# Attention and two expert layers on one core: another order of the transfers that SyncE issues in a head

## The chip, the cores and the metric

The kernel runs on 1 core of one Trainium2 chip. The metric is the device time of one execution in microseconds. The kernel before takes 752.03 us (median of 3 runs, 750.96 to 754.53).

## What is computed

All arrays are f32. Three stages follow each other; the output of one is the input of the next.

```python
# 1. attention, 16 heads (2 x 8) of 768 positions x 64
q_bucket = sum((q @ proj > 0) * 2**arange(6)); k_bucket likewise
mask     = q_bucket[:, None] == k_bucket[None, :]
scores   = where(mask, q @ k.T / 8, -1e9); scores -= max(scores, -1)
attn     = exp(scores); attn /= sum(attn, -1) + 1e-9
x        = attn @ v                        # 1536 tokens x 512 after the heads are joined
# 2. dense layer, w_in 512 x 2048, w_out 2048 x 512
h = x @ w_in; g = where(h > 0, h, exp(min(h, 0)) - 1); x = g @ w_out
# 3. 8 experts (512 x 1024, 1024 x 512), one for each token; tokens with x @ w_skip <= 0 pass unchanged
out = x + gate * (relu(x @ w1[e]) @ w2[e])
```

## The kernel before, in words

Precision comes from splitting each f32 operand into a rounded high part and the rest (`hi`, `lo`; `p_hi`, `p_lo`; `W[:, j, 0..3, :]`), so that most products take three matmuls or two stacked ones.

**A head on TensorE.** `scores(h, s)` (L1187) makes six tiles of transposed scores, s = 0 to 5; four tiles later `weighted(n, b)` (L1199) multiplies the probabilities of tile n with v. Between them PE prepares the next heads, by the plan of `head_units` (L59): in head h the six row maxima `MAX` of head h+1 (L1180), at s = 2 the transposes `T` of q and k of head h+2 (L1164), at s = 3 the transpose of the maxima, at s = 4 the hash bits. `scores(h, 0)` waits for `neg_copied` (L1192): the row of minus maxima of head h must have been copied by DMA from `minus_max` into row 96 of `q_hi_rows_T` (`copy_minus_maxima`, L342).

**SyncE (SP)** issues nearly all transfers from one in-order queue, and its waits hold up all that is behind them. The loop at L386 runs over the heads h:

- `load_qk(h+3)` (two transfers of 192 KB) and `load_v(h+2)` (192 KB); the first waits for the transposes of head h+1, the second for `v_ready` (POOL's `low_of_v`, L504);
- in odd heads from 3: `store_rden` (12 inverse sums per partition to `den_rows` in HBM, L355), `load_w` of one dense tile (two transfers of 256 KB, L321), and `load_rden` (L361), which waits until the store has landed and reads the inverse sums back as `rden_rows`, each of 2 rows of 3 KB spread over 64 partitions, 384 KB;
- `copy_rows(h+2)` (four copies of 64 partitions x 3 KB within SBUF, L327; waits for `hi_done` of head h+2, that is ACT's `round_qk` behind the transposes), `copy_minus_maxima(h+1)`, `copy_low_rows(h+2)` (two more copies);
- in even heads from 2: `load_den` (L347), the sums of the pair of heads before.

The broadcast is written with the two rows as its leading dimension:

```python
sp.dma_start(rden_rows[:, :], den_rows[2 * pair:2 * pair + 2, :].unsqueeze(1).broadcast_to([2, D, S]))
```

**GpSimd (POOL)** makes the low parts of four tiles of six (`low_probs`, L512), the low part of v, in even heads from 4 `normalise(h // 2 - 2)` (L532: waits for `rden_loaded`, two multiplications into `attn_T`), in odd heads 3 to 9 `split_w` of one dense tile (L521), in heads 11 and 13 half of `split_x` (L543). All in program order: per head low_probs of 6h-2, 6h-1 and 6h, then normalise or the splits, then low_probs of 6h+3 (L571), then low_of_v. **VectorE (DVE)** has the other two tiles, the row maxima, `inverse_den` (L875) and, in the dense layer, `low_of_w` (L918). **ScalarE (ACT)** has the exponentials, `high_probs`, `outputs` (L687) and `high_of_w` (L721).

**Dense layer.** Four blocks of 384 tokens; each goes over 16 tiles j of `W` (`up`, L1238; `down`, L1251). Block 0 runs while the later tiles are still loaded and split. The tiles of `W` overlay the attention buffers: 4 to 7 are free after the last scores, 8 to 12 after `od_ready` of head 15, 13 to 15 after the last normalise (`xt_ready`). So SP (L405 to L416) loads 4 to 7, then `load_den(7)`, tile 8, `store_rden(7)`, `load_rden(7)`, tiles 9 to 12, and then 13 to 15. Four semaphores `w_loaded` go round: tile j waits until tile j-4 has been split (`w_done` of j-3).

Of the kernel before, what the change touches and what calls it, by code (L numbers as in the profile page):

```python
# [15 lines left out]
P = 128  # L16
B, NH, S, D = 2, 8, 768, 64
HEADS = B * NH
# [25 lines left out]


EARLY = 4

# [28 lines left out]
def build(nc, q, k, v, proj, w_in, w_out, w_skip, w_gate, w1, w2, out, y_rows):  # L78
    ctx = ExitStack()
    with ctx:  # L80
# [14 lines left out]
        def sem(name):  # L95
            return ctx.enter_context(nc.semaphore(name))
# [4 lines left out]
        w_raw = [sb(f"w_raw{j}", [P, 4, 512], F32, at=W_at + j * W_TILE)[0] for j in range(FT)]  # L101
# [134 lines left out]
        s_ = {n: sem(n) for n in names}  # L236
        qk_loaded = [sem(f"qk_loaded{u}") for u in range(2)]
        v_loaded = [sem(f"v_loaded{u}") for u in range(2)]
        rows_copied = [sem(f"rows_copied{i}") for i in range(3)]
        w_loaded = [sem(f"w_loaded{i}") for i in range(4)]  # L240
        e_loaded = [sem(f"expert_loaded{i}") for i in range(4)]
        gathered = [sem(f"rows_gathered{i}") for i in range(EXPERTS)]
        scattered = [sem(f"rows_scattered{i}") for i in range(2)]
# [4 lines left out]
        w_in_v = w_in.rearrange("(c p) (j f) -> j p c f", p=P, f=P)  # L248
# [60 lines left out]
        def _(sp):  # L309
            def load_qk(h):  # L310
                if h >= 2:
                    sp.wait_ge(s_["tq_done"], h - 1)
                for i, x in enumerate((q_h, k_h)):
                    sp.dma_start(qk_nat[h % 2][:, :, i, :], x[h]).then_inc(qk_loaded[h % 2], 16)

            def load_v(h):
                if h >= 2:
                    sp.wait_ge(s_["v_ready"], h - 1)
                sp.dma_start(v_nat[h % 2][:, :, :], v_h[h]).then_inc(v_loaded[h % 2], 16)

            def load_w(j):  # L321
                if j >= 4:
                    sp.wait_ge(s_["w_done"], j - 3)
                sp.dma_start(w_raw[j][:, 1, :].rearrange("p (c f) -> p c f", f=P), w_in_v[j]).then_inc(w_loaded[j % 4], 16)
                sp.dma_start(w_raw[j][:, 3, :], w_out_v[j]).then_inc(w_loaded[j % 4], 16)

            def copy_rows(h):  # L327
                i = h % 3
# [26 lines left out]
            def store_rden(pair):  # L355
                sp.wait_ge(s_["rden_ready"], pair + 1)
                for u in range(2):
                    sp.dma_start(den_rows[2 * pair + u].rearrange("(p t) -> p t", t=QT), rden[:, u * QT:(u + 1) * QT])\
                        .then_inc(s_["rden_stored"], 16)

            def load_rden(pair):  # L361
                sp.wait_ge(s_["rden_stored"], 32 * (pair + 1))
                if pair:
                    sp.wait_ge(s_["xt_ready"], pair)
                sp.dma_start(rden_rows[:, :], den_rows[2 * pair:2 * pair + 2, :].unsqueeze(1).broadcast_to([2, D, S]))\
                    .then_inc(s_["rden_loaded"], 16)
# [17 lines left out]
            copy_minus_maxima(0)  # L384

            for h in range(HEADS):  # L386
                if h + 3 < HEADS:
                    load_qk(h + 3)
                if h + 2 < HEADS:
                    load_v(h + 2)  # L390
                if h % 2 and h >= 3:
                    store_rden(h // 2 - 1)
                    if h // 2 <= EARLY:
                        load_w(h // 2 - 1)
                    load_rden(h // 2 - 1)
                if h + 2 < HEADS:
                    copy_rows(h + 2)
                if h + 1 < HEADS:
                    copy_minus_maxima(h + 1)
                if h + 2 < HEADS:  # L400
                    copy_low_rows(h + 2)
                if h % 2 == 0 and h:
                    load_den(h // 2 - 1)

            sp.wait_ge(s_["st_done"], QT * HEADS)  # L405
            for j in range(EARLY, EARLY + 4):
                load_w(j)
            load_den(PAIRS - 1)
            load_w(EARLY + 4)
            store_rden(PAIRS - 1)  # L410
            load_rden(PAIRS - 1)
            for j in range(EARLY + 5, 13):
                load_w(j)
            sp.wait_ge(s_["xt_ready"], PAIRS)
            for j in range(13, FT):
                load_w(j)  # L416
# [49 lines left out]
        def _(pool):  # L466
# [53 lines left out]

            def split_w(j):  # L521

                pool.wait_ge(w_loaded[j % 4], 32 * (j // 4 + 1))
                for i, raw in enumerate((1, 3)):
                    pool.tensor_scalar(W[:, j, 2 * i, :], w_raw[j][:, raw, :], 1.0, 1.0, ALU.mult, ALU.mult)\
                        .then_inc(s_["w_step"], 1)
                    pool.wait_ge(s_["w_step"], 2 * j + i + 1)
                    low = pool.tensor_tensor(W[:, j, 2 * i + 1, :], w_raw[j][:, raw, :], W[:, j, 2 * i, :].bitcast(F32),
                                             ALU.subtract)
                low.then_inc(s_["w_done"], 1)  # L530
# [29 lines left out]
            for h in range(HEADS):  # L560
                if h:
                    low_probs(QT * h - 2)
                    low_probs(QT * h - 1)
                low_probs(QT * h)
                if h % 2 == 0 and h >= 4:
                    normalise(h // 2 - 2, *low_ready(QT * h))
                if h % 2 and h >= 3 and h // 2 <= EARLY:
                    split_w(h // 2 - 1)
                if h in (11, 13):
                    split_x(0, ((h - 11) // 2,))  # L570
                low_probs(QT * h + 3)  # L571
                if 0 < h < HEADS - 1:
                    low_of_v(h + 1)
# [78 lines left out]
        def _(act):  # L652
# [67 lines left out]

            def high_of_w(j):  # L721

                act.wait_ge(w_loaded[j % 4], 32 * (j // 4 + 1))
                act.activation(W[:, j, 0:4:2, :], w_raw[j][:, 1:4:2, :], ACT.Copy).then_inc(s_["w_high"], 1)

            def g_high(n, j):
# [73 lines left out]
        def _(dve):  # L800
# [134 lines left out]
            def block_body(n):  # L935
                first = isinstance(n, int)
                for j in range(FT):
                    dve.wait_ge(s_["e_ready"], n * FT + (j + 1))

                    reached(dve, "gl_ready", n * FT + (j - 1))  # L940
                    dve.scalar_tensor_tensor(gb[:, j % 2, :], e_neg[:, j % 2, :], -1.0, banks[:, j % 2, 0:BN],  # L941
                                             ALU.add, ALU.max).then_inc(s_["g_ready"], 1)
                    if first and j == 1:
                        dve.wait_ge(s_["pv_done"], QT * HEADS)
                    if j:
                        g_low(n, j - 1)
                    elif not first:
                        g_low(n - 1, FT - 1)
                    if first and EARLY <= j + 2 < FT:
                        low_of_w(j + 2)  # L950
                    if first and j == 4:
                        inverse_den(PAIRS - 1)
                    if not first:
                        if j == 2:
                            y_T_copy(n - 1, 0)
                            y_T_copy(n - 1, 1)
                        elif j == 3:
                            y_T_copy(n - 1, 2)
                        elif j == 4:
                            logits_copy(n - 1)  # L960
# [476 lines left out]
```

## Time and profile before

| | before |
|---|---|
| median of 3 runs | 752.03 us (750.96 to 754.53) |
| profiled execution, its own time | 749.8 us |
| its span, first to last instruction | 747.8 us |
| mean granted TensorE clock | 0.944 of full |
| PE busy | 658.4 us (88%) |
| DVE, ACT, POOL busy | 344.3, 328.2, 252.1 us |
| head 4 to the end of attention | 96 to 327 us |
| dense layer | 327 to 610 us |
| experts | 636 to 748 us |

PE is TensorE's matmuls, PEld its weight loads, SPq SyncE's queue as issuer of DMAs. An engine's idle time before an instruction is shown with what released it. The clock column of a window is the share of 2.4 GHz that was granted; 0.50 is the lower level, 1.2 GHz.

### The profile page before, as it was taken

What the parts mean: (1) busy time and instruction counts of PE and PEld (TensorE: products, weight loads), DVE (VectorE), ACT (ScalarE), POOL (GpSimd) and SP (SyncE); (2) the same over time, 40 slices, a digit from 0 to 9 for tenths busy, and PEclk for the clock granted to TensorE, in tenths of its full rate; (3) what the DMA queues carried; (4) which work ended last, traced back from release to release, by engine and by line L of the source; (5) the groups of instructions that cost most, each with busy time, mean ns of one, the idle gap of its engine ahead of it and who ended that gap; (6) DMA issues with size and microseconds to landing.
All of it is one profiled execution on the core that took longest, in us unless ns stands there. A gap on an engine that the chain in (4) does not pass through costs nothing.

```text
span 747.8 us, 9851 instructions
## 1 busy us (share of the span) xinstructions
PE 658.4 (88%) x3632; PEld 610.3 (82%) x3632; DVE 344.3 (46%) x495; ACT 328.2 (44%) x505; POOL 252.1 (34%) x204
## 2 busy tenths in 40 slices
PE   4799688695959696999799999999999994999996
PEld 3699688695959595998699999999999983999986
DVE  6766656372737374425452322322232225654642
ACT  2367557373737464756354233333333331234340
POOL 4044747464657465672203000300001202711211
PEclk9999989797979798999899999999999996899999
DMA  7344626163453523041500100200036675599300
GB/s 177 87 122 122 150 65 156 40 170 69 130 110 97 116 76 85 3 134 53 166 29 34 53 1 0 84 0 0 0 140 224 241 267 209 192 372 354 134 11 22
DMA packets 68151, 84.04 MB, mean 112 GB/s; under 512 B 34356, under 2 KB 44692, under 8 KB 68112
## 3 DMA queue, kind: packets, MB, share of 16 engines
q1 hardware_dynamic: 66832, 79.88, 36.2%
q0 software_dynamic: 1280, 3.65, 1.4%
q8 instruction: 24, 0.39, 0.2%
q14 instruction: 15, 0.12, 0.1%
HBM read 56.64 MB, written 8.44 MB: 87 GB/s over the span
## 4 chain that ended last, share of the span: by engine, by line
PE 73%; DMA 15%; DVE 4%; SPq 3%; issue 2%; ACT 2%; POOL 0%; POOLq 0%; DVEq 0%; ACTq 0%
PE banks L1247 17%; PE banks L1258 16%; DMA q_hi_rows_T<-minus_max 9%; PE banks L1371 8%; PE banks L1386 6%; PE banks L1180 4%; PE banks L1195 4%; PE banks L1196 3%; PE banks L1211 3%; PE banks L1212 3%; PE banks L1213 3%; SPq L334 2%; DVE row_max L848 2%; DMA w_raw<-in_moe_w_out 2%; DMA y_rows<-y 2%
## 5 line engine op out<-in xcount | busy, mean ns | idle before, releaser
L1247 PE MATMUL banks<-x_hi,w_split 128*128 (+1 forms) x512 | 143.1, 340 | 4.1 <-DVE w_split L920 4.1
L517 POOL TENSOR_TENSOR probs_lo<-probs,probs_hi 128x768 fp32r<-128x768 f32 x64 | 107.6, 1691 | 110.5 <-ACT probs_hi L684 107.3
L848 DVE TENSOR_REDUCE row_max<-banks 128x1 f32<-128x768 f32 x96 | 88.5, 957 | 110.0 <-PE banks L1180 110.0
L676 ACT ACTIVATE probs<-banks 128x768 f32<-128x768 f32 x96 | 77.9, 811 | 121.4 <-PE banks L1196 120.5
L941 DVE SCALAR_TENSOR_TENSOR g<-exp_min_h,banks 128x384 f32<-128x384 f32 x64 | 35.5, 554 | 191.0 <-ACT exp_min_h L746 191.0
L1258 PE MATMUL banks<-w_split,g_hi 128*128 128x512 f32 x384 | 121.0, 396 | 0.1
L1195 PE MATMUL banks<-q_lo_hi_T,k_hi_lo_T 128*128 128x384 f32 x192 | 72.4, 377 | 54.6 <-DMA q_hi_rows_T<-minus_max 46.6
L743 ACT ACTIVATE exp_min_h<-banks 128x384 f32<-128x384 f32 x64 | 31.5, 492 | 169.8 <-PE banks L1247 169.8
L1247 PEld LDWEIGHTS banks<-x_hi,w_split 128*128 128x128 f32 x512 | 94.7, 190 | 7.1 <-issue 4.5
L1195 PEld LDWEIGHTS banks<-q_lo_hi_T,k_hi_lo_T 128*128 128x128 f32 x192 | 38.6, 201 | 61.5 <-issue 48.9
L1247 PE MATMUL banks<-x_lo,w_split 128*128 (+1 forms) x256 | 86.7, 339 | 0.0
L1258 PEld LDWEIGHTS banks<-w_split,g_hi 128*128 128x128 f32 x384 | 71.2, 189 | 12.4 <-DVE g_lo L915 0.5
L684 ACT ACTIVATE probs_hi<-probs 128x768 fp32r<-128x768 f32 x96 | 80.4, 838 | 0.0
L1258 PE MATMUL banks<-w_split,g_lo 128*128 128x512 f32 x192 | 76.2, 397 | 0.0
L1211 PE MATMUL banks<-probs_hi,v_hi_ones 128*128 128x386 f32 x192 | 67.3, 350 | 1.8 <-ACT o_and_den L695 1.8
L1196 PE MATMUL banks<-q_hi_rows_T,k_hi_rows_T 128*128 128x384 f32 x192 | 68.2, 355 | 0.0
L1212 PE MATMUL banks<-probs_lo,v_hi_ones 128*128 128x386 f32 x192 | 67.1, 350 | 0.0
L1213 PE MATMUL banks<-probs_hi,v_lo_zeros 128*128 128x386 f32 x192 | 67.0, 349 | 0.0
L1371 PEld LDWEIGHTS banks<-x_T,expert_w 128*128 128x128 f32 x512 | 59.9, 196 | 1.9 <-issue 1.3
L1371 PE MATMUL banks<-x_T,expert_w 128*128 128x128 f32 x512 | 60.1, 279 | 0.9 <-DVE x_T L1059 0.9
L1180 PE MATMUL banks<-k_hi_rows_T,q_hi_rows_T 96*128 96x384 f32 x192 | 55.3, 379 | 2.4 <-DMA k_hi_lo_T<-qk_lo_T 1.9
L1247 PEld LDWEIGHTS banks<-x_lo,w_split 128*128 128x128 f32 x256 | 48.6, 190 | 2.6
(161 smaller groups left out, 1023.5 us busy)
## 6 DMA issues: line engine op xcount, KB each, us to landing
expert_w<-in_moe_w SPq DMA_DIRECT2D x32, 1024.0 KB, 6.2
w_raw<-in_moe_w_in SPq DMA_DIRECT2D x16, 256.0 KB, 3.9
w_raw<-in_moe_w_out SPq DMA_DIRECT2D x16, 256.0 KB, 4.4
qk_nat<-in_q SPq DMA_DIRECT2D x16, 192.0 KB, 3.5
qk_nat<-in_k SPq DMA_DIRECT2D x16, 192.0 KB, 3.6
v_nat<-in_v SPq DMA_DIRECT2D x16, 192.0 KB, 3.3
q_hi_rows_T<-qk_hi_T SPq DMA_DIRECT2D x16, 192.0 KB, 2.7
k_hi_rows_T<-qk_hi_T SPq DMA_DIRECT2D x16, 192.0 KB, 3.0
```

Of the source, the lines that this page charges most:

```text
L517: pool.tensor_tensor(p_lo[:, n % RING, :, 0:HALF], probs[:, n % RING, :].rearrange("p (b n) -> p b n", b=2), p_hi[:, n % RING, :, 0:HALF]. ...
L684: act.activation(p_hi[:, n % RING, :, 0:HALF], probs[:, n % RING, :].rearrange("p (b n) -> p b n", b=2), ACT.Copy).then_inc(s_["p_hi_ready ...
L848: dve.tensor_reduce(mx[:, t:t + 1], psum("MAX", h, t), AX.XY, ALU.max).then_inc(s_["max_done"], 1)
L1180: mm = pe.matmul(to[:, b, :], qb[h % 3][0:NEG_ROW, i * P:i * P + P], kb[h % 3][0:NEG_ROW, b * HALF:b * HALF + HALF], start=True, stop=True)
L1195: pe.matmul(to[:, b, :], ka[i][:, s * P:s * P + P], qa[i][:, half], start=True, stop=False)
L1196: mm = pe.matmul(to[:, b, :], kb[i][:, s * P:s * P + P], qb[i][:, half], start=False, stop=True)
L1211: pe.matmul(to, v_hi[h % 2][:, t, :], high, start=(t == 0), stop=False)
L1212: pe.matmul(to, v_hi[h % 2][:, t, :], low, start=False, stop=False)
L1213: mm = pe.matmul(to, v_lo[h % 2][:, t, :], high, start=False, stop=(t == QT - 1))
L1247: mm = pe.matmul(banks[:, j % 2, 0:BN], w, x, start=(c == 0 and w is hi and x is x_hi), stop=(c == KC - 1 and w is lo))
L1258: mm = pe.matmul(banks[:, 2 + t, :], g, W[:, j, part, :], start=(j == 0 and i == 0), stop=(j == FT - 1 and i == 2))
L1371: mm = pe.matmul(banks[:, j // 4, j % 4 * P:j % 4 * P + P], w1_sb[:, r, c, j * P:j * P + P], xeT[:, e % 2, c, :], start=(c == 0), stop=(c ...
```

## The change

SP's loop over the heads begins with `copy_rows(h+2)`, `copy_minus_maxima(h+1)`, `copy_low_rows(h+2)` and `load_den`; `load_qk(h+3)` and `load_v(h+2)` follow; then in even heads 4 to 10 `load_w(h // 2 - 2)`, in odd heads `store_rden` and `load_rden`. There are eight signals `w_loaded` in place of four, so a tile waits for the split of the tile eight before it. POOL's `split_w` and `split_x` come one pair of heads later. Behind the heads, tiles 9 and 10 are loaded ahead of `store_rden(7)` and 11 and 12 ahead of `load_rden(7)`; the inverse of the last sums moves from j = 4 to j = 3 of block 0.

```diff
@@ -44,6 +44,7 @@
 
 
 EARLY = 4
+W_AHEAD = 8
 
 
 
@@ -237,7 +238,7 @@
         qk_loaded = [sem(f"qk_loaded{u}") for u in range(2)]
         v_loaded = [sem(f"v_loaded{u}") for u in range(2)]
         rows_copied = [sem(f"rows_copied{i}") for i in range(3)]
-        w_loaded = [sem(f"w_loaded{i}") for i in range(4)]
+        w_loaded = [sem(f"w_loaded{i}") for i in range(W_AHEAD)]
         e_loaded = [sem(f"expert_loaded{i}") for i in range(4)]
         gathered = [sem(f"rows_gathered{i}") for i in range(EXPERTS)]
         scattered = [sem(f"rows_scattered{i}") for i in range(2)]
@@ -319,10 +320,10 @@
                 sp.dma_start(v_nat[h % 2][:, :, :], v_h[h]).then_inc(v_loaded[h % 2], 16)
 
             def load_w(j):
-                if j >= 4:
-                    sp.wait_ge(s_["w_done"], j - 3)
-                sp.dma_start(w_raw[j][:, 1, :].rearrange("p (c f) -> p c f", f=P), w_in_v[j]).then_inc(w_loaded[j % 4], 16)
-                sp.dma_start(w_raw[j][:, 3, :], w_out_v[j]).then_inc(w_loaded[j % 4], 16)
+                if j >= W_AHEAD:
+                    sp.wait_ge(s_["w_done"], j - W_AHEAD + 1)
+                sp.dma_start(w_raw[j][:, 1, :].rearrange("p (c f) -> p c f", f=P), w_in_v[j]).then_inc(w_loaded[j % W_AHEAD], 16)
+                sp.dma_start(w_raw[j][:, 3, :], w_out_v[j]).then_inc(w_loaded[j % W_AHEAD], 16)
 
             def copy_rows(h):
                 i = h % 3
@@ -384,15 +385,6 @@
             copy_minus_maxima(0)
 
             for h in range(HEADS):
-                if h + 3 < HEADS:
-                    load_qk(h + 3)
-                if h + 2 < HEADS:
-                    load_v(h + 2)
-                if h % 2 and h >= 3:
-                    store_rden(h // 2 - 1)
-                    if h // 2 <= EARLY:
-                        load_w(h // 2 - 1)
-                    load_rden(h // 2 - 1)
                 if h + 2 < HEADS:
                     copy_rows(h + 2)
                 if h + 1 < HEADS:
@@ -401,16 +393,26 @@
                     copy_low_rows(h + 2)
                 if h % 2 == 0 and h:
                     load_den(h // 2 - 1)
+                if h + 3 < HEADS:
+                    load_qk(h + 3)
+                if h + 2 < HEADS:
+                    load_v(h + 2)
+                if h % 2 == 0 and 4 <= h < 4 + 2 * EARLY:
+                    load_w(h // 2 - 2)
+                if h % 2 and h >= 3:
+                    store_rden(h // 2 - 1)
+                    load_rden(h // 2 - 1)
 
             sp.wait_ge(s_["st_done"], QT * HEADS)
             for j in range(EARLY, EARLY + 4):
                 load_w(j)
             load_den(PAIRS - 1)
-            load_w(EARLY + 4)
+            for j in range(EARLY + 4, 11):
+                load_w(j)
             store_rden(PAIRS - 1)
+            for j in range(11, 13):
+                load_w(j)
             load_rden(PAIRS - 1)
-            for j in range(EARLY + 5, 13):
-                load_w(j)
             sp.wait_ge(s_["xt_ready"], PAIRS)
             for j in range(13, FT):
                 load_w(j)
@@ -520,7 +522,7 @@
 
             def split_w(j):
 
-                pool.wait_ge(w_loaded[j % 4], 32 * (j // 4 + 1))
+                pool.wait_ge(w_loaded[j % W_AHEAD], 32 * (j // W_AHEAD + 1))
                 for i, raw in enumerate((1, 3)):
                     pool.tensor_scalar(W[:, j, 2 * i, :], w_raw[j][:, raw, :], 1.0, 1.0, ALU.mult, ALU.mult)\
                         .then_inc(s_["w_step"], 1)
@@ -564,10 +566,10 @@
                 low_probs(QT * h)
                 if h % 2 == 0 and h >= 4:
                     normalise(h // 2 - 2, *low_ready(QT * h))
-                if h % 2 and h >= 3 and h // 2 <= EARLY:
-                    split_w(h // 2 - 1)
-                if h in (11, 13):
-                    split_x(0, ((h - 11) // 2,))
+                if h % 2 and 5 <= h < 5 + 2 * EARLY:
+                    split_w(h // 2 - 2)
+                if h in (13, 15):
+                    split_x(0, ((h - 13) // 2,))
                 low_probs(QT * h + 3)
                 if 0 < h < HEADS - 1:
                     low_of_v(h + 1)
@@ -720,7 +722,7 @@
 
             def high_of_w(j):
 
-                act.wait_ge(w_loaded[j % 4], 32 * (j // 4 + 1))
+                act.wait_ge(w_loaded[j % W_AHEAD], 32 * (j // W_AHEAD + 1))
                 act.activation(W[:, j, 0:4:2, :], w_raw[j][:, 1:4:2, :], ACT.Copy).then_inc(s_["w_high"], 1)
 
             def g_high(n, j):
@@ -948,7 +950,7 @@
                         g_low(n - 1, FT - 1)
                     if first and EARLY <= j + 2 < FT:
                         low_of_w(j + 2)
-                    if first and j == 4:
+                    if first and j == 3:
                         inverse_den(PAIRS - 1)
                     if not first:
                         if j == 2:
```

## Rows read from the trace of the kernel before

**Rows 1.** The page: the chain that ended last, shares by line.

```profile
PE banks L1247 17%; PE banks L1258 16%; DMA q_hi_rows_T<-minus_max 9%; PE banks L1371 8%; PE banks L1386 6%; PE banks L1180 4%; PE banks L1195 4%; PE banks L1196 3%; PE banks L1211 3%; PE banks L1212 3%; PE banks L1213 3%; SPq L334 2%; DVE row_max L848 2%; DMA w_raw<-in_moe_w_out 2%; DMA y_rows<-y 2%
```

**Rows 2.** Waits: engine, line, releaser: us in total, times, longest.

```profile
PE banks L1195 <- DMA q_hi_rows_T<-minus_max: 46.6, 7, 8.4
```

**Rows 3.** Timeline of PE: start, us, instruction [idle before it, releaser].

```profile
96.38 0.66 PE L1195 MATMUL banks<-q_lo_hi_T,k_hi_lo_T 128*128 128x384 f32 x1 [8.28 <-DMA q_hi_rows_T<-minus_max]
...
116.64 0.33 PE L1211 MATMUL banks<-probs_hi,v_hi_ones 128*128 128x386 f32 x1
...
298.56 0.66 PE L1195 MATMUL banks<-q_lo_hi_T,k_hi_lo_T 128*128 128x384 f32 x1 [6.62 <-DMA q_hi_rows_T<-minus_max]
...
367.68 0.66 PE L1247 MATMUL banks<-x_hi,w_split 128*128 128x384 f32 x1 [4.06 <-DVE w_split L920]
```

**Rows 4.** Windows behind seven restarts: us; PE, PEld, DVE, ACT, POOL busy; clock; DMA share; GB/s.

```profile
96.40:100.30 3.90, 3.90 (x12) 3.90 (x13) 0.66 (x1) 1.54 (x2) 0.65 (x1) 0.50 0.06 16
...
367.70:373.30 5.60, 5.60 (x16) 5.28 (x17) 2.23 (x4) 1.38 (x4) 0.86 (x7) 0.50 0.58 187
sum 30.90, PE 30.88 PEld 30.58 DVE 7.45 ACT 10.58 POOL 5.93; mean PE 4.41 PEld 4.37 DVE 1.06 ACT 1.51 POOL 0.85
```

**Rows 5.** Chain in order of time: start, us, what.

```profile
84.37 11.87 DMA q_hi_rows_T<-minus_max
...
287.85 10.57 DMA q_hi_rows_T<-minus_max
```

**Rows 6.** Timeline of SP, the queue that issues: start, us, transfer.

```profile
79.40 0.59 SPq L365 DMA_DIRECT2D rden_rows<-den_rows  x1
81.87 0.54 SPq L334 DMA_DIRECT2D q_hi_rows_T<-qk_hi_T  x1
...
107.37 0.52 SPq L334 DMA_DIRECT2D q_hi_rows_T<-qk_hi_T  x1
...
122.61 0.53 SPq L334 DMA_DIRECT2D q_hi_rows_T<-qk_hi_T  x1
...
239.99 0.81 SPq L358 DMA_DIRECT2D den_rows<-rden  x2
242.05 0.58 SPq L365 DMA_DIRECT2D rden_rows<-den_rows  x1
...
282.74 0.59 SPq L365 DMA_DIRECT2D rden_rows<-den_rows  x1
285.37 0.52 SPq L334 DMA_DIRECT2D q_hi_rows_T<-qk_hi_T  x1
...
338.93 1.15 SPq L353 DMA_DIRECT2D den<-o_and_den  x2
```

**Rows 7.** Windows of DMA traffic, columns as in rows 4.

```profile
83.00:88.40 5.40, 4.82 (x26) 4.50 (x26) 4.25 (x5) 4.06 (x7) 5.31 (x4) 1.00 0.98 223
292.50:295.00 2.50, 0.00 (x0) 0.00 (x0) 0.00 (x0) 0.38 (x1) 2.05 (x2) 0.96 0.13 50
295.00:298.00 3.00, 0.00 (x0) 0.00 (x0) 0.00 (x0) 0.00 (x0) 0.58 (x1) 0.50 0.13 34
```

**Rows 8.** Timeline of POOL.

```profile
111.41 1.70 POOL L517 TENSOR_TENSOR probs_lo<-probs,probs_hi 128x768 fp32r<-128x768 f32 x1 [1.81 <-ACT probs_hi L684]
114.62 1.01 POOL L509 TENSOR_TENSOR v_lo_zeros<-v_nat,v_hi_ones 128x384 fp32r<-128x384 f32 x1 [1.52 <-ACT v_hi_ones L669]
...
329.97 3.84 POOL L538 TENSOR_TENSOR attn_T<-o_and_den,rden_rows 64x768 f32<-64x768 f32 x2
...
362.71 3.73 POOL L538 TENSOR_TENSOR attn_T<-o_and_den,rden_rows 64x768 f32<-64x768 f32 x2 [22.31 <-DMA rden_rows<-den_rows]
```

**Rows 9.** Chain in block 0, in order of time: start, us, what.

```profile
352.26 11.64 DMA w_raw<-in_moe_w_out
```

**Rows 10.** The page, DMA issues: KB each, median us from issue to landing.

```profile
w_raw<-in_moe_w_out SPq DMA_DIRECT2D x16, 256.0 KB, 4.4
```

**Rows 11.** The instructions of tile qk_nat: issue to landing.

```profile
DMA to landing us min/median/max: 3.1/3.5/11.3
```

## The prediction

> **What bounds the kernel now.** I read the chain that ended last first. It is TensorE work nearly throughout, with one entry that is none: the transfer of the minus maxima, 9% of the span [rows 1]. The waits say who pays: the first scores of a head wait 46.6 us for it, in seven places [rows 2]. The timeline of PE places six of them at the starts of heads 4, 6, 8, 10, 12 and 14. They last 8.28, 8.42, 8.26, 8.14, 6.50 and 6.62 us, 46.2 us in all; the first and last stand in the rows. A seventh stall, of 4.06 us, comes in block 0 of the dense layer, where PE waits for the split of a late weight tile [rows 3]. Elsewhere in the heads PE runs nearly without gaps. Behind each of the seven restarts the granted clock is 0.50 (1.2 GHz) for 3.1 to 5.8 us, 30.9 us together, 5.6 of them in block 0 [rows 4]. Work done there takes twice its time, so 25.3 / 2 = 12.6 us go in the heads and 2.8 in block 0.
>
> **Why that transfer is late.** It carries 3 KB and takes 11.87 us from its issue; before head 14 it takes 10.57 [rows 5]. SP shows what is ahead of it in odd heads: `load_rden`, issued 2.5 us before the row copies (79.40 and 81.87, 282.74 and 285.37) [rows 6]. Once the other traffic is over, a DMA share of 0.13 moves 50 GB/s, then 34 [rows 7]. 0.13 of 16 is two engines, 25 GB/s each. The broadcast's leading dimension is 2, so I read it as 192 KB on each of two engines, with the pieces of everything issued later queued behind it there. While row copies use all engines, 223 GB/s flow, 14 on each [rows 7]. The Trainium skill says the same in "DMA: Bandwidth & Descriptors", Rules for kernel authors: a leading dimension of size c confines a transfer to c engines; by that rule the order of issue cannot cure it, and the trace agrees.
>
> Does this account for the measured delay? Count from R, the issue of the row copies, before head 14. Traffic lags issue by 1.2 us (estimate), so the broadcast starts at R - 1.4, the copies at R + 1.1. Per slow engine: 196 KB of broadcast, 2.5 us alone x 25 = 63 KB, 5.4 us beside the copies x 14 = 75 KB, the other 58 KB in 2.3 us; then its 49 KB of rows at 17 GB/s (34 over two), 2.9 us; landing about 1.4. Sum 1.1 + 5.4 + 2.3 + 2.9 + 1.4 = R + 13.1. Measured: 287.85 + 10.57 - 285.37 = 13.05 [rows 5, 6]. PE began to wait at R + 6.2 (head 4) and R + 6.6 (head 14) [rows 3, 6]; I take 6.3, and 0.1 for the restart.
>
> **Order within the loop.** The loop is cyclic. Copies, maximum row, low copies are followed by q, k, v before and after; what they name moves by one head. The new text "copies first" therefore puts nothing new ahead of the maxima. What changes is that the inverse sums travel behind the copies of an odd head, so before those of the next even head, and that the weights are no longer in that gap. The stall moves to the starts of heads 5, 7, 9, 11 and 13, and the question is how far ahead of the copies the broadcast now starts.
>
> **Lead of the broadcast.** Successive row copies are 15.24 us apart when nothing stalls (107.37, 122.61) [rows 6]. In an odd head SP issues copies, maximum row and low copies in 4.6 us, q, k and v in 1.6, without v's wait, since the needed low part of v is now a head old. The stores are issued at R + 6.2. Their data queue behind six copies (1.18 MB at 223 GB/s, 5.3 us), q, k (about 2) and v (about 1), so they land at about R + 10.5, and the broadcast is issued at 10.7 and starts at 11.9. The next copies start at 15.24 + 1.1 = 16.3: a lead of 4.4 us, where it was 2.5 (about 1.3 behind weights). Now 110 KB go alone, 75 beside the copies, 11 remain (0.4 us). The maximum row lands at 1.1 + 5.4 + 0.4 + 2.9 + 1.4 = R' + 11.2, and the stall is 11.2 + 0.1 - 6.3 = 5.0 us.
> Bounds: if the stores found an empty queue, the broadcast would be issued 2.06 us after them, as at 239.99 to 242.05 [rows 6], at R + 8.3: lead 6.8, all of it done beside the copies, stall about 1.7. With no more lead than 2.5, 6.9. I take 5.0, worked from the queue's bytes.
>
> **POOL.** `normalise` now finds its data late. The broadcast lands at R' + 1.1 + 5.4 + 0.4 + 1.4 = 8.3; two multiplications take 3.84 and low_probs of tile 6h+3 1.70 [rows 8], ready at 13.8. PE needs that tile at R' + 9.3 without a stall (116.64 - 107.37) [rows 3, 6], with the stall of 5.0 at 14.3. So this wait is hidden, by 0.5 us, under the maximum's; if that cover goes, it takes its place. Low v costs 1.01 and further tiles 1.7 each against PE's 2.5 per tile, so POOL catches up. The weights' split, one pair later, sits behind them in odd heads with nearly a head of slack; half of split_x goes to head 15: nothing on the path, up to 1 us at worst.
> After head 13 no row copies follow. The broadcast starts at R + 11.9 and ends 7.9 later; the last maximum row lands near 21.2 against a need near 20 (stall 1.2), but POOL is free of normalise only near 25 and low_probs near 26.7, where PE, now 1.77 us a tile, wants it near 23.5: 3.2 more, 0.9 for the next. Together 5.3.
>
> **Sum for the heads.** 46.2 - 5 x 5.0 - 5.3 = 15.9 us. Clock: a shorter stall may or may not bring the 1.2 GHz. Bounds are 0 and all 12.6 us; the nearest row, the 6.62 us stall, still brought 3.1 us of it [rows 3, 4], so I take 2 us of gain.
>
> **Loads moved.** q and k of head h+3 are issued one head later than before, at R + 5 to 6; landing has a median of 3.5 us [rows 11], and the transposes come about 13 us behind R: hidden in odd heads. In even heads they queue behind the slow pair; the worst landing before, 11.3 us [rows 11], gives R' + 17.5, and with the stall the transposes come at about 18. Hidden, barely. In heads 0 to 3 there is no broadcast: nothing.
>
> **Block 0.** Before, tile 9 was issued behind the last broadcast, took 11.64 us, and was late [rows 9]. Now tiles 8 to 10 go at 340 to 343, right behind `load_den(7)` (338.93) [rows 6], and 11 and 12 before the broadcast. Eight signals let them; tile 12 waits for tile 4's split, done by 342. Each weight half lands in 4.4 us at the median [rows 10], some 10 us before its use. The broadcast is issued near 348 and lands near 359, normalise ends near 363 (it ended at 366.4 [rows 8]), tiles 13 to 15 land from 367, and up(13) comes near 376. The stall of 4.06 us and its 2.8 us of clock go: 6.9 us. The earlier inverse is one 0.23 us instruction on an idle stretch of DVE.
>
> **Total** 15.9 + 2 + 6.9 = 24.8 us. The profiled execution took 749.8 (span 747.8), so 725.0 by it; it is 2.2 under the median, and against the median of 752.03 the forecast is 727.2.
>
> **Rivals.**
> A, the forecast: stalls move and shorten. With its bounds (stalls of 1.7 to 6.9, clock 12.6 to 0) 697 to 741. Chance 0.55.
> B, the broadcast is over before the next copies, and all head stalls go, with their clock: 752.0 - 46.2 - 12.6 - 6.9 = 686. For it: 15.24 us between copies leave room for 7.9 us alone if the stores landed at once. Against: the bytes in the queue. Chance 0.15. The Trainium skill, same page, Anatomy of one DMA, fits 2.0 us + bytes / 436 GB/s, 2.9 us for 393 KB; by that B would hold. The trace speaks against it here, with two engines at 50 GB/s.
> C, the broadcast is as close to the copies as before: the stalls only change heads, and block 0 alone pays: 752.0 - 6.9 = 745. Chance 0.2.
> D, slower: SP stands in `load_rden` waiting for the stores, with the row copies of the next head behind it. If the stores took 11.3 us, as the slowest loads did [rows 11], SP would come free at R + 17.5, 2.3 us late; broadcast and copies would start together. 1.1 + 2.3 + 5.4 + (196 - 75 - 10) / 25 = 4.4 + 2.9 + 1.4 give R' + 17.5, stalls of 11.3: 5 x 11.3 + 10 = 66.5 against 46.2, less 6.9: about 765. It turns slower than before when a stall passes 9.5 us. In favour: a store in front of a wait; against: its measured 2.06 us. Chance 0.05.
> E, nothing: in a cyclic loop the new order is the old one, and block 0 finds another late tile: 752. Chance 0.05.
>
> **Numbers.** A change of 0.5%, 3.8 us, is about what a measurement can tell. A, B and C are faster: 0.90; E 0.05 same; D 0.05 slower. The range leaves out B and D: from A's lower part to C, 702 to 745.5. A's own range is 697 to 741.
>
> **What the profile would show.** Right: waits for the minus maxima at heads 5 to 13 and not at even ones, about 5 us each; `load_rden` issued about 11 us behind an odd head's copies, two-engine stretches in even heads; POOL waiting for `rden_rows` in every even head; no wait for w_split in block 0. Wrong: no such stalls (B), old lengths (C), SP late at the copies (D), or waits of the transposes for q and k.

## The result, and the profile after

| | before | after |
|---|---|---|
| median (4 runs each, same chip) | 751.91 us | 719.84 us (716.7 to 721.86) |
| ratio | | 0.9564, 95% interval 0.9519 to 0.9609 |
| profiled execution, its own time | 749.8 us | 721.02 us |
| its span | 747.8 us | 719.0 us |
| mean granted TensorE clock | 0.944 | 0.958 |

Faster by 32 us; forecast were 727.2 and a range of 702 to 745.5, under case A (the stalls move by a head and shorten). In the four later sets of runs the kernel before had medians of 748.3 to 749.2 us, so some 3 us of the 32 may belong to this set.

The page of the changed kernel, the chain that ended last, shares by line:

```profile
PE banks L1249 19%; PE banks L1260 18%; PE banks L1373 8%; PE banks L1388 6%; DMA q_hi_rows_T<-minus_max 6%; PE banks L1182 4%; PE banks L1197 4%; PE banks L1198 3%; PE banks L1213 3%; PE banks L1215 3%; PE banks L1214 3%; DVE row_max L850 3%; SPq L335 2%; DMA y_rows<-y 2%; DMA rden_rows<-den_rows 1%
```

Its waits: us in total, times, longest:

```profile
POOL attn_T L540 <- DMA rden_rows<-den_rows: 72.1, 7, 18.9
...
PE banks L1197 <- DMA q_hi_rows_T<-minus_max: 24.1, 6, 5.7
...
PE banks L1197 <- DVE qk_lo_T L830: 9.8, 14, 1.3
```

Its timeline of PE, the instructions that followed idle time:

```profile
107.66 0.66 PE L1197 MATMUL banks<-q_lo_hi_T,k_hi_lo_T 128*128 128x384 f32 x1 [5.65 <-DMA q_hi_rows_T<-minus_max]
...
146.33 0.66 PE L1197 MATMUL banks<-q_lo_hi_T,k_hi_lo_T 128*128 128x384 f32 x1 [5.15 <-DMA q_hi_rows_T<-minus_max]
...
184.58 0.66 PE L1197 MATMUL banks<-q_lo_hi_T,k_hi_lo_T 128*128 128x384 f32 x1 [5.18 <-DMA q_hi_rows_T<-minus_max]
...
221.27 0.41 PE L1197 MATMUL banks<-q_lo_hi_T,k_hi_lo_T 128*128 128x384 f32 x1 [4.01 <-DMA q_hi_rows_T<-minus_max]
...
257.59 0.66 PE L1197 MATMUL banks<-q_lo_hi_T,k_hi_lo_T 128*128 128x384 f32 x1 [3.64 <-DMA q_hi_rows_T<-minus_max]
...
293.56 0.44 PE L1213 MATMUL banks<-probs_hi,v_hi_ones 128*128 128x386 f32 x1 [0.85 <-POOL probs_lo L519]
...
296.18 0.44 PE L1213 MATMUL banks<-probs_hi,v_hi_ones 128*128 128x386 f32 x1 [0.61 <-POOL probs_lo L519]
```

The six stalls at the starts of even heads, 46.2 us, are gone [rows 3]. Five stand at the starts of heads 5, 7, 9, 11 and 13 instead, 23.6 us together, and in head 15 there are 1.5 us for POOL's low probabilities. That is 21.1 us less. The maximum row's share of the chain fell from 9% to 6% [rows 1]. The wait of the transposed scores' first matmul for `qk_lo_T` grew from 7.9 to 9.8 us.

Its timeline of SP around the copies of heads 3 and 4 of the loop:

```profile
80.49 0.53 SPq L335 DMA_DIRECT2D q_hi_rows_T<-qk_hi_T  x1
...
86.40 0.63 SPq L320 DMA_DIRECT2D v_nat<-in_v  x1
87.07 0.91 SPq L359 DMA_DIRECT2D den_rows<-rden  x2
91.51 0.58 SPq L366 DMA_DIRECT2D rden_rows<-den_rows  x1
96.17 0.54 SPq L335 DMA_DIRECT2D q_hi_rows_T<-qk_hi_T  x1
```

The chain in order of time, two of the five transfers of the maximum row:

```profile
98.78 8.74 DMA q_hi_rows_T<-minus_max
...
250.54 6.92 DMA q_hi_rows_T<-minus_max
```

The broadcast leaves 11.0 us behind the copies of its head and 4.66 ahead of the next ones; before, the distance was 2.5 [rows 6]. In the four later pairs it leaves 9.6 to 10.8 us behind and 4.96 to 6.04 ahead; the next pair is an example. The maximum row takes 8.74 us where it took 11.87 [rows 5].

```profile
128.91 0.57 SPq L366 DMA_DIRECT2D rden_rows<-den_rows  x1
134.91 0.53 SPq L335 DMA_DIRECT2D q_hi_rows_T<-qk_hi_T  x1
```

Windows of the changed kernel: two of the five around the restarts and the sum of the five (where one begins ahead of its restart, PE's busy time is what counts), then one of block 0 (columns as in rows 4):

```profile
106.10:112.90 6.80, 5.24 (x16) 5.27 (x17) 1.33 (x2) 1.54 (x2) 6.48 (x5) 0.50 0.42 124
...
256.30:263.10 6.80, 5.51 (x17) 5.54 (x18) 1.61 (x2) 1.54 (x2) 6.49 (x6) 0.50 0.31 75
...
sum 27.20, PE 21.62 PEld 21.71 DVE 4.95 ACT 7.72 POOL 26.25; mean PE 4.32 PEld 4.34 DVE 0.99 ACT 1.54 POOL 5.25
...
325.00:350.00 25.00, 25.00 (x127) 22.64 (x126) 15.99 (x19) 14.18 (x25) 6.95 (x13) 1.00 0.40 121
```

21.6 us of PE's work still run at 0.50, so 10.8 us go there where 12.6 went. In this stretch of block 0, where the late tile would have been waited for, PE is busy throughout at the full clock; the stall of 4.06 us and its slow stretch are gone.

**Sum.** 21.1 (stalls) + 1.8 (clock) + 6.9 (block 0) - 1.9 (`qk_lo_T`) = 27.9 of the 28.8 us between the profiled executions; 0.9 is not accounted for.

### The profile page after: what moved, and what is told of

It is laid out like the page before. It is cut to its first block, busy times and chain, and to the rows that moved or that the text cites. A ratio compares the mean times of both kernels' runs of the same rounds, so it can differ in the third digit from the quotient of the medians.

```text
span 719.0 us, 9850 instructions
## 1 busy us (share of the span) xinstructions
PE 653.2 (91%) x3632; PEld 605.7 (84%) x3632; DVE 342.5 (48%) x495; ACT 327.9 (46%) x505; POOL 245.9 (34%) x204
## 4 chain that ended last, share of the span: by engine, by line
PE 76%; DMA 11%; DVE 5%; SPq 3%; issue 2%; ACT 1%; POOL 1%; POOLq 0%; DVEq 0%; ACTq 0%
PE banks L1249 19%; PE banks L1260 18%; PE banks L1373 8%; PE banks L1388 6%; DMA q_hi_rows_T<-minus_max 6%; PE banks L1182 4%; PE banks L1197 4%; PE banks L1198 3%; PE banks L1213 3%; PE banks L1215 3%; PE banks L1214 3%; DVE row_max L850 3%; SPq L335 2%; DMA y_rows<-y 2%; DMA rden_rows<-den_rows 1%
## 5 line engine op out<-in xcount | busy, mean ns | idle before, releaser
L540 POOL TENSOR_TENSOR attn_T<-o_and_den,rden_rows 64x768 f32<-64x768 f32 x16 | 30.2, 1885 | 72.8 <-DMA rden_rows<-den_rows 72.1
```

## The experiments

Each ran beside the kernel before on the same chip; ratios are to it, with 95% intervals. The chip differs from set to set, so kernels of different sets are compared by their ratios. Each stall list is from the profiled run's timeline of PE.

**Is the wide broadcast the cure, and what is the order worth then?** Both kernels, with the broadcast cut in two transfers of 64 partitions:

```diff
-sp.dma_start(rden_rows[:, :], den_rows[2 * pair:2 * pair + 2, :].unsqueeze(1).broadcast_to([2, D, S]))
+for u in range(2):
+    sp.dma_start(rden_rows[u * D:u * D + D, :], den_rows[2 * pair + u:2 * pair + u + 1, :].broadcast_to([D, S]))
 ...
```

> The changed kernel, with the broadcast of the inverse sums cut in two transfers of 64 partitions each, whose leading dimension is 64 and no longer 2; bytes, order and waits are kept. Theory 1 (192 KB on each of two DMA engines hold up the maximum row behind them): the five stalls at heads 5 to 13 (23.6 us in the profile), the two waits for POOL in head 15 (1.5) and the 1.2 GHz behind the stalls (about 10) all go, 719.8 - 35 = 685 us; POOL waits for the inverse sums under 3 us a head. Theory 2 (the sum of all bytes in an even head holds the maximum row up, whichever engines carry them): the same bytes, so no more than 3 us, 717 to 720.

> The kernel before, with the same cut of the broadcast alone. Theory 1: all six head stalls (46.2 us), their clock (12.6) and the stall of block 0 with its clock (6.9) go without any change of order, 751.9 - 65.7 = 686 us, the same as the changed kernel with the cut; so the change is worth nothing once the broadcast is wide. Theory 2: the order is what counts, so the stalls stay near 7 us each and the time above 740.

Measured: 688.02 us, 0.9214 (0.917 to 0.9259), in the changed kernel, and 689.12 us, 0.9219 (0.9187 to 0.9251), in the kernel before. The head stalls are gone in both, and in the kernel before the wait of block 0 for `w_split` is gone too, though its order is the old one. In the wide version of the changed kernel the broadcast carries this traffic:

```profile
94.40:97.20 2.80, 2.80 (x20) 2.76 (x19) 2.16 (x3) 1.65 (x3) 1.09 (x1) 1.00 0.51 143
```

and the list of DMA issues says, for one of the two parts (KB, median us to landing):

```profile
rden_rows<-den_rows SPq DMA_DIRECT2D x16, 192.0 KB, 3.5
```

The two parts, issued 0.6 us apart, land within some 4 us, where POOL began 13.2 us behind the issue in the changed kernel (91.51 to 104.73). So the stalls were the broadcast on two engines. That it is now two transfers instead of one is not the cure: cut in two but on four engines, it keeps two thirds of the stalls (further down). Once it is wide, the new order is worth nothing that can be measured: the ratios differ by 0.0005. The Trainium skill, "DMA: Bandwidth & Descriptors", Rules for kernel authors, says that an outermost dimension of size c below 16 confines a transfer to at most c engines; the cure follows it. The trace agrees: the share of 0.51 is 8 of 16 engines on the mean of that stretch, where the broadcast with two in front showed 0.13, two engines [rows 7].

**Which part of the change pays?** The end alone (tiles 8 to 10 ahead of the last stores, 11 and 12 ahead of the last broadcast, eight signals, the last inverse at j = 3), and the loop alone:

```diff
 # the end alone; the loop alone is the rest of the change
-load_w(EARLY + 4)
+for j in range(EARLY + 4, 11):
+    load_w(j)
 store_rden(PAIRS - 1)
-load_rden(PAIRS - 1)
-for j in range(EARLY + 5, 13):
+for j in range(11, 13):
     load_w(j)
+load_rden(PAIRS - 1)
 ...
```

> The kernel before, with only what the change does behind the heads: eight weight signals, tiles 9 to 12 loaded ahead of the last broadcast, the last inverse at j = 3. Forecast: the 4.06 us stall of block 0 and its 2.8 us of clock go, 745 us, and the six head stalls stay as they were. Rival: another tile is late in its place, 750 or more.

> The kernel before, with only the new order in SP's loop and the splits of weights and x one pair later on POOL, four weight signals and the old order behind the heads. Forecast: the rest of the gain, 719.8 + 6.9 = 727 us; head stalls as in the changed kernel (3.6 to 5.7 us at heads 5 to 13), and a stall of about 4 us in block 0 as before. Rival: the two parts overlap, and the sum of their gains is not the whole: below 722 or above 732.

Measured: the end 743.13 us, 0.992 (0.9891 to 0.995), with no stall in block 0 and six head stalls of 6.69 to 9.59 us; the loop 723.74 us, 0.9689 (0.9657 to 0.9721), with stalls of 3.60, 4.55, 4.74, 3.32 and 2.58 us and the one of block 0 (4.44 us) kept. 0.992 x 0.9689 = 0.961 against the whole change's 0.956, with overlapping intervals: the parts add up as far as can be told. Up to head 15 the loop alone is the changed kernel's loop, yet its stalls are 3.60 to the other's 5.65, and so on: one profiled stall is good to 1 or 2 us.

**Which move within the loop pays?** Three moves, each alone in the kernel before. First q, k and v, then the weights (their split on POOL a pair later), then stores and broadcast:

```diff
 # e9: q, k, v behind the low copies
-if h + 3 < HEADS: load_qk(h + 3)
-if h + 2 < HEADS: load_v(h + 2)
 store_rden, load_w, load_rden in odd heads
 copy_rows, copy_minus_maxima, copy_low_rows, load_den
+if h + 3 < HEADS: load_qk(h + 3)
+if h + 2 < HEADS: load_v(h + 2)
 # e10: weights to the ends of the even heads
-if h // 2 <= EARLY: load_w(h // 2 - 1)
+if h % 2 == 0 and 4 <= h < 4 + 2 * EARLY: load_w(h // 2 - 2)
 # e12: stores and broadcast to the end of the odd heads
-store_rden(h // 2 - 1)
-load_rden(h // 2 - 1)
 copy_rows, copy_minus_maxima, copy_low_rows
+if h % 2 and h >= 3: store_rden(h // 2 - 1); load_rden(h // 2 - 1)
```

> The kernel before with one edit: in even heads q, k and v of the next pair go behind the row copies of low_logits (from head 2 on) instead of ahead of them; weights, maximum row, stores and broadcast stay where they were. Theory 1 (the gain came from issuing the store ahead of the load of the broadcast's successor, that is from the broadcast's distance to the next copies): within 0.5% of before, 745 to 752 us, and the six waits for the maximum row stay at 6 to 9 us in heads 4 to 14. Theory 2 (the copies gain by being first in the even half): the copies are ahead of 384 KB that they stood behind, and the time falls by 10 us or more, to below 738.

> The kernel before with the weights' loads moved from the odd heads 3 to 13, where they stood ahead of the broadcast's landing and the next copies, to the ends of the even heads 4 to 10; nothing else moves. Theory 1 (the stalls of before are the broadcast on two engines, lengthened by the weights that share them): heads 4 to 10 fall from 8.3 us each to about the 6.6 us of heads 12 and 14, 7 us in all, near 741 and a ratio of 0.991. Theory 2 (weights do not matter to the stall): ratio 1.0 within 0.005. Theory 3 (the weights were the main thing in the way): stalls of 3 us or less, below 725.

> The kernel before with one edit: in odd heads the stores and the broadcast go behind the low copies instead of ahead of q_hi's row copies; q, k, v, the weights and the end of the loop stay where they were. If the whole gain of the loop's new order is the broadcast's distance to the next copies, this edit alone gives it: stalls in heads 5 to 13 of 3.5 to 5.5 us, within 5 us of the 724 of the loop's new order as a whole, a ratio of 0.965 to 0.975, and the 4 us stall in block 0 stays. If the order of the three parts only works together (weights or loads would eat the distance), stalls stay above 6.5 us and the ratio above 0.985.

Measured: q, k, v 748.75 us, 0.9997 (0.9965 to 1.003), with six stalls of 6.4 to 8.4 us. The edit moves the loads in every head, not only in the even ones of which the expectation speaks. The loads alone do nothing: in the cyclic loop they are behind the maximum row either way.

Weights: 748.08 us, 0.9988 (0.9968 to 1.0007), stalls of 7.97, 8.13, 7.51, 7.02, 6.88 and 6.37 us, 43.9 in all. My 7 us did not come. (The weights stood in the odd heads 3 to 9, not up to 13, and their split on POOL moved with them, which the expectation leaves out.) Its timeline of SP shows that the gap stayed short:

```profile
115.89 1.51 SPq L358 DMA_DIRECT2D den_rows<-rden  x2
119.34 0.58 SPq L365 DMA_DIRECT2D rden_rows<-den_rows  x1
121.12 0.53 SPq L334 DMA_DIRECT2D q_hi_rows_T<-qk_hi_T  x1
```

The weights are out of it, but SP now comes to 3.45 us from store to broadcast, and the broadcast leaves 1.8 us ahead of the copies; in the other pairs it is 2.3 to 2.8 (before: 2.1 to 3.3).

Stores and broadcast: 723.34 us, 0.966 (0.9623 to 0.9697), with stalls of 3.35, 2.42, 2.92, 3.33 and 2.77 us in heads 5 to 13, and 3.89 us in block 0. By the ratios this one move is the loop's whole gain. Its timeline of SP:

```profile
85.62 1.95 SPq L358 DMA_DIRECT2D den_rows<-rden  x2
89.45 0.60 SPq L365 DMA_DIRECT2D rden_rows<-den_rows  x1
90.11 0.61 SPq L314 DMA_DIRECT2D qk_nat<-in_q  x1
90.76 3.37 SPq L314 DMA_DIRECT2D qk_nat<-in_k  x1
...
97.19 0.53 SPq L334 DMA_DIRECT2D q_hi_rows_T<-qk_hi_T  x1
```

**Does the stall follow the broadcast's distance to the next copies?** Two ways to enlarge it in the changed kernel: q, k, v back ahead of the row copies, so that they come behind the broadcast; or only the stores ahead of q, k, v.

```diff
 # e5
+if h + 3 < HEADS: load_qk(h + 3)
+if h + 2 < HEADS: load_v(h + 2)
 copy_rows, copy_minus_maxima, copy_low_rows, load_den
-if h + 3 < HEADS: load_qk(h + 3)
-if h + 2 < HEADS: load_v(h + 2)
 # e6
+if h % 2 and h >= 3: store_rden(h // 2 - 1)
 load_qk, load_v, load_w
-if h % 2 and h >= 3: store_rden(h // 2 - 1)
 load_rden
```

> The changed kernel with q, k and v put back to the head of the loop, before the row copies; everything else as changed. So in an odd head the stores of the inverse sums and the broadcast come right behind the low copies, ahead of q, k and v. Theory 1 (only the broadcast's lead over the next row copies counts): lead 8.1 us in place of 4.4, stalls at the odd heads of about 2.3 us (3.6 to 5.7 now), 703 us. Theory 2 (what the change says: copies and maximum row have to come ahead of the loads): the stalls are back at 7 us or more, above 735.

> The changed kernel with only the stores of the inverse sums moved ahead of q, k and v in odd heads; the broadcast stays behind v. Theory 1: the stores no longer queue behind the bytes of q, k and v, the broadcast is issued about 7.5 us behind the copies (it was 9.7 to 11.0), lead 6.7, stalls about 1.7 us, 699 us. Theory 2 (the stores' own landing is what takes the time): issue time as before, no change from 719.8.

Measured: q, k, v first 718.43 us, 0.9588 (0.9521 to 0.9655), neither number; stalls of 4.85, 5.20, 3.70, 5.52 and 4.25 us. The distance did grow, to 96.24 - 88.41 = 7.8 us, but the loads now stand in it, on the slow engines too:

```profile
88.41 0.59 SPq L366 DMA_DIRECT2D rden_rows<-den_rows  x1
89.04 0.61 SPq L315 DMA_DIRECT2D qk_nat<-in_q  x1
90.10 3.12 SPq L315 DMA_DIRECT2D qk_nat<-in_k  x1
93.28 2.53 SPq L320 DMA_DIRECT2D v_nat<-in_v  x1
96.24 0.53 SPq L335 DMA_DIRECT2D q_hi_rows_T<-qk_hi_T  x1
```

So a distance with the loads in it is worth no more than the changed kernel's shorter one without them; in the run that moves stores and broadcast alone the distance is 7.7 us, also with the loads in it, and it gained no more than the loop's whole new order either. What counts is the distance less what is queued in it. The stores first, 704.2 us, 0.9397 (0.9322 to 0.9471), with stalls of 2.88, 2.09, 2.25, 2.21 and 2.24 us, show it:

```profile
85.92 1.08 SPq L359 DMA_DIRECT2D den_rows<-rden  x2
...
88.39 0.64 SPq L320 DMA_DIRECT2D v_nat<-in_v  x1
89.07 0.58 SPq L366 DMA_DIRECT2D rden_rows<-den_rows  x1
96.55 0.55 SPq L335 DMA_DIRECT2D q_hi_rows_T<-qk_hi_T  x1
```

Here no load is issued in the 7.5 us (7.5 to 8.1 over the five pairs), and the stall is 2.3 us on the mean against 4.7 in the changed kernel, where the distance is 4.7 to 6.0. The forecast of 1.7 us a stall was too low.

**Does POOL's normalise come next?** The changed kernel with the wide broadcast, issued only in the next even head, behind the maximum row and low copies, so that it delays no maximum:

```diff
 copy_low_rows(h + 2)
+if h % 2 == 0 and h >= 4: load_rden(h // 2 - 2)
 ...
 store_rden(h // 2 - 1)
-load_rden(h // 2 - 1)
+if h == HEADS - 1: load_rden(h // 2 - 1)
```

> The changed kernel with the wide broadcast (16 engines), but issued in the next even head behind the low copies, so that it lands about 10 us behind those copies and blocks nobody's transfer. The stalls for the maximum row stay away. If POOL's wait for the inverse sums inside its order is the next bound (low parts of tile 6h+3 queued behind normalise), PE waits for POOL once a pair instead, 10 + 3.8 + 1.7 - 9.3 = about 6 us each at odd heads: 688 + 6 x 6 = 724 us and some clock. If POOL has slack I did not see, it stays at 688 to 692.

Measured: 729.72 us, 0.975 (0.9684 to 0.9816). No stall for a maximum; PE waits for POOL in its place, six times, 29.8 us (5.30, 5.20, 5.02, 5.43, 5.03, 3.79). Its timelines of PE and then of POOL:

```profile
111.49 0.69 PE L1217 MATMUL banks<-probs_hi,v_hi_ones 128*128 128x386 f32 x1 [5.30 <-POOL probs_lo L523]
```

```profile
105.85 3.67 POOL L544 TENSOR_TENSOR attn_T<-o_and_den,rden_rows 64x768 f32<-64x768 f32 x2 [11.59 <-DMA rden_rows<-den_rows]
109.76 1.67 POOL L523 TENSOR_TENSOR probs_lo<-probs,probs_hi 128x768 fp32r<-128x768 f32 x1 [0.24 <-POOL attn_T L544]
```

Counted from the row copies at 96.77, the tile is ready at 14.7 us, nearly as in the changed kernel (14.2, below), but PE, which nothing stopped before, comes for it at 9.4. A POOL as late as that, which cost nothing in heads 5 to 13 under the maximum's stall, costs 5 us a pair without this cover. With the wide broadcast issued at its old place PE waits for POOL nowhere and for a maximum 0.5 us at most.

**Four engines.** The kernel before, each half of the broadcast as [4, 16, 768]:

```diff
-den_rows[2 * pair:2 * pair + 2, :].unsqueeze(1).broadcast_to([2, D, S])
+den_rows[2 * pair + u:2 * pair + u + 1, :].unsqueeze(1).broadcast_to([4, D // 4, S])  # u = 0, 1
```

> The kernel before with the broadcast spread over four engines (two transfers with a leading dimension of 4), 96 KB on each. The sum by bytes: heads 4, 6, 8 and 10 stall 3.9 us, 12 and 14 2.1 (6.5 to 8.4 with two engines, about 0.3 with sixteen); block 0 does not stall; 748 - 26 - 4 of clock - 7 = about 711 us, ratio 0.95. If the number of engines did not matter beyond two, or mattered as a threshold, it would be either 748 or 689.

Measured: 730.99 us, 0.9744 (0.9664 to 0.9824), against 711; stalls of 5.80, 5.13, 5.23, 6.47, 3.87 and 4.04 us, 30.5 where I had worked out 19.8, and 2.51 in block 0. Windows of this kernel, broadcast alone and then beside the copies:

```profile
81.90:82.90 1.00, 1.00 (x7) 0.98 (x6) 1.00 (x2) 1.00 (x3) 0.45 (x1) 1.00 0.29 97
...
83.50:88.50 5.00, 4.85 (x26) 4.53 (x26) 4.01 (x5) 3.63 (x7) 4.92 (x4) 1.00 1.03 199
```

Alone it moves twice what two engines did, 97 GB/s. Beside the copies all queues together give 199 GB/s where before they gave 223 [rows 7]. That and the stall's size go together; why the mixture is slower was not settled.

**Both cures together.** The changed kernel with the wide broadcast, and with the stores ahead of q, k, v:

> The changed kernel with both edits that helped it: the broadcast in two transfers of 64 partitions, and the stores of the sums ahead of q, k and v. With the wide broadcast alone TensorE waited 0.7 us in all for the maximum row, so there is nothing left that the earlier store could give back: 688 us within 2 us, the same as the wide broadcast alone. If the distance still mattered, it would be faster by 3 us or more.

Measured: 687.62 us, 0.9199 (0.9171 to 0.9228), the same as the wide broadcast alone. Both beat both kernels: by 8% the kernel before, by 4% the changed one.

## Why the prediction was right

**The bound and its cause.** Right: a broadcast confined to two engines, with the maximum row queued behind it. The wide versions take the stalls away, and leave 688 where rival B, all head stalls gone, was priced at 686. That "the order of issue cannot cure it" holds only in part: no order took the stalls away, but the stores ahead of the loads brought them from 4.7 to 2.3 us each. Rival B leant on 2.9 us for the broadcast, an estimate from the Trainium skill, "DMA: Bandwidth & Descriptors", Anatomy of one DMA. That section gives its fit for transfers issued by GpSimd, and SyncE issues this one, so it was no support for B. Here the broadcast took 10.41 us from issue to landing with little else to carry (277.27, below).

**Order within the loop.** Right: "copies first" is worth nothing (0.9997), and the place of the broadcast is what pays (0.966 by that move alone). I counted the weights' leaving the gap in with it; alone it gives nothing measurable.

**Lead and stall.** The lead was put at 4.4 us in transfers' starts, from stores issued at R + 6.2 and the broadcast at R + 10.7. Measured are R + 6.6 and 11.0 at head 3, with a lead of 4.66 in issues. The maximum row was to land at R' + 11.2: it did at 98.78 + 8.74 - 96.17 = R' + 11.35. PE began to wait 0.5 us earlier than taken, at 107.66 - 5.65 - 96.17 = R' + 5.8; in the four later pairs it was R' + 6.2 to 6.3, as taken. Stalls of 5.0 each, 25.0, were forecast; 5.65 to 3.64, 23.6, came. That the mean fits so well is in part luck. In heads 7, 11 and 13 the distance was 6.0 us, for which the prediction's own sum gives a stall of about 3.2 (148 KB alone, 48 and the rows beside the copies, 1.1 + 3.4 + 3.5 + 1.4 = R' + 9.4); measured are 5.15, 4.01 and 3.64. The lead was longer than forecast, and a given lead bought less. Part of it is the estimate of 1.2 us from issue to traffic: at head 5 the slow pair's traffic sets in at 93.4, 1.9 us behind the issue of 91.51. The 1.4 us for landing stand in no row either: in the kernel before the slow pair's traffic runs until 298.4, and the maximum row lands at 298.42. What they stand for in the sum is open. Why those of heads 11 and 13 are shorter is open; in the kernel before heads 12 and 14 were so too, and moving the weights did not level them.

**The last pair.** Wrong in size, and the largest miss: 5.3 us forecast, 1.5 measured. The step that failed is "starts at R + 11.9", which took the odd head's full queue. In head 13 of the loop there are no q and k left to load (`load_qk(16)` is past the last head), so the stores had less in front of them, and the broadcast went out at R + 8.0 (269.27 to 277.27) instead of R + 10.7. SP's timeline, then the chain:

```profile
269.27 0.53 SPq L335 DMA_DIRECT2D q_hi_rows_T<-qk_hi_T  x1
...
273.76 0.59 SPq L320 DMA_DIRECT2D v_nat<-in_v  x1
274.39 0.94 SPq L359 DMA_DIRECT2D den_rows<-rden  x2
277.27 0.58 SPq L366 DMA_DIRECT2D rden_rows<-den_rows  x1
```

```profile
277.27 10.41 DMA rden_rows<-den_rows
```

It landed at R + 18.4 instead of 21.2. No stall for a maximum came, and the tile of low probabilities was ready at R + 24.2 instead of 26.7.

**POOL.** Right that it is hidden in heads 5 to 13. The timelines of POOL and then of PE in the changed kernel's head 5:

```profile
104.73 3.68 POOL L540 TENSOR_TENSOR attn_T<-o_and_den,rden_rows 64x768 f32<-64x768 f32 x2 [11.02 <-DMA rden_rows<-den_rows]
108.65 1.68 POOL L519 TENSOR_TENSOR probs_lo<-probs,probs_hi 128x768 fp32r<-128x768 f32 x1 [0.24 <-POOL attn_T L540]
```

```profile
113.27 0.33 PE L1213 MATMUL banks<-probs_hi,v_hi_ones 128*128 128x386 f32 x1
```

The tile is ready at R' + 14.2 (forecast 13.8), and PE came for it at R' + 17.1, not at 14.3, since its work behind the restart ran at the lower clock; the margin was 2.9 us and not 0.5, by a slowness that the forecast had not counted. The late broadcast shows what the cover was worth. POOL's seven waits for `rden_rows`, 72.1 us, cost the 1.5 us in head 15.

**Loads moved.** Priced at nothing, and no transpose waited; the slowest landing of q and k fell from 11.3 to 7.1 us [rows 11]. Not forecast: `qk_lo_T` is 1.9 us later in sum.

**Clock.** 2 us forecast, 1.8 measured: in the profiled execution of the changed kernel the shorter stalls still bring the lower level behind each. That is not so in every execution. In the loop alone PE restarts behind 3.60 us and stays at the full clock:

```profile
107.55 0.41 PE L1195 MATMUL banks<-q_lo_hi_T,k_hi_lo_T 128*128 128x384 f32 x1 [3.60 <-DMA q_hi_rows_T<-minus_max]
```

```profile
107.60:113.60 6.00, 6.00 (x34) 5.87 (x35) 3.73 (x5) 3.19 (x5) 5.76 (x5) 1.00 0.43 125
```

So do two of the five stalls with the stores first (2.25 and 2.24 us) and two with the broadcast moved alone (2.42 and 2.92). That the forecast of 2 us was met is thus partly a matter of which execution was profiled.

**Block 0.** 6.9 us forecast; the end alone gave 0.8% of 748, 6.0 us, with an interval of 3.7 to 8.2.

**Sum.** 24.8 forecast against 28.8 between the profiled executions: 3.8 from the last pair, 1.4 from the five stalls, 0.9 not accounted for, less 1.9 (`qk_lo_T`) and 0.2 (clock). The medians differ by 3.3 us more than the profiled executions do: the one of before was 2.1 under its median, the one of after 1.2 over.

**The other cases' prices.** By its own terms, with the last pair at 5.3, case A spans 700 to 739 and not 697 to 741. Case D puts 10 us for the last pair without a source; with it the change turns slower from stalls of 8.6 us on, and the 9.5 given belongs to 5.3. Neither bears on the forecast.

## What to carry to other kernels

A few KB can be late by the whole length of a large transfer issued before them, if that one sits on few engines (3 KB took up to 11.87 us here): compare the share of DMA busy with the GB/s in a stretch where it runs alone, and widen it before moving it about; here the new order gave 4.4%, the shape 8%, and with the shape the order gave nothing more. When the order must do it, count the time between the narrow transfer and the next critical one less the bytes queued in between. And look at the loop's last iterations separately: some of what is queued in front of a step is missing there.

## What the hardware did that was not expected

- Where k of the next head is issued behind the two-engine broadcast, SP's own issue takes 3.12 and 3.37 us instead of 0.65 to 0.7 us, v's 2.53. With the wide broadcast k's takes 0.74 us at most, in either kernel, so it is the narrow broadcast that lengthens it. I read it as a full queue that also holds up the engine that issues; this reading is argued and not shown.
- Four engines instead of two took away a third of the stalls, not the 57% that the sum by bytes gave; sixteen took away all. Beside the copies 199 GB/s flowed, fewer than with the narrower broadcast (223).
- In the changed kernel a stall of 3.64 us brings the lower clock for as long (5.5 us of work) as one of 5.65 us (5.2 us), and those of 4.01 and 5.18 us for 3.4 us each. In other runs stalls of 2.2 to 3.6 us brought none. So the length of a stall alone does not give its price.
